# Attention in a fused kernel: six shared PSUM banks, turned groups of a pair in one run, new written-out orders of work

## The chip, the cores and the metric

The kernel runs on one core of a Trainium2 chip. The metric is the device time of one execution in microseconds (us); lower is better.

## What is computed

Three blocks follow one another: windowed attention, a mixture of four attention experts, and a gated block that mixes tokens. The change touches the first and the seam to the second. Cut to what matters:

```python
batch, n_heads, seq, head_dim = (2, 8, 768, 64)
n_sink, window = (4, 128)
scores = scale * np.matmul(q, k.transpose(0, 1, 3, 2))
keep = is_sink | in_window            # in_window: 0 <= i - j < 128
scores = np.where(keep, scores, -1000000000.0)
a = np.exp(scores - np.max(scores, axis=-1, keepdims=True))
a = a / (np.sum(a, axis=-1, keepdims=True) + 1e-09)
x = np.matmul(a, v)                   # then _moe_ref, then _moe2_ref
```

## The kernel before, in words

**Attention.** The 16 heads are worked as 8 pairs. Two heads of a pair lie on the two halves of the partitions, so that the scores of both run side by side in TensorE. The 768 rows of queries are six tiles (t = 0 to 5) of 128. Since the window is 128 wide, a tile meets only its own block of keys, the block before it and the 4 sinks: 260 columns, 132 for tile 0. For each pair and tile these steps follow one another:

- TensorE makes the scores of both heads in two PSUM banks (`score_tile`, L1017).
- VectorE (DVE) adds the mask, takes the row maximum and moves the tile to SBUF in `Pa` (`mask_tile`, L697).
- ScalarE (ACT) takes the exponential and the row sums (`exp_tile`, L511).
- DVE inverts the sums of the whole pair (`invert_sums`, L720 and L722).
- GpSimd (POOL) scales the probabilities in six groups, one for each head h and each group g of two tiles, and gathers the sinks' columns (`scale_pair`, L417 and L419; `gather_sinks`, L428).
- TensorE transposes ("turns") each group into a bank (`turn_group`, L1034; 3 transposes for group 0, 4 for the others) and the gathered sinks (`turn_sinks`, L1048).
- ACT and DVE copy the turned groups to `PTa` (`copy_group`, L521 and L708), three each; DVE copies the sinks (`copy_sinks`, L714).
- TensorE multiplies with the values (`weigh_pair`, L1066) and adds the sinks' part (`weigh_sinks`, L1076), into banks 6 and 7.
- ACT takes the sums out (`take_x`, L529 and L531), DVE the low part (`x_low`, L727).

**Banks.** Scores use banks 0 to 3 (a few tiles of the first pairs banks 4 to 7), turned groups alternate between banks 4 and 5 (`A_TURN`), sums lie in 6 and 7, and the turned sinks in a free part of bank 7.

**Order.** Every engine works its steps in program order and waits on semaphores. The orders are written out in loops at the end of each engine's part. TensorE's loop over pairs p is: scores of pair p+1 tiles 0 and 1, weighing of pair p-1, tiles 2 and 3, sinks of p-1, two turned groups of p, tile 4, two groups, tile 5, two groups, sinks of p turned. In the last pair the first two projections of the experts (`project`, L991 to L993) take the place of tiles 4 and 5, and projections 2 and 3 stand behind the sinks. At the start, `keep_busy` (L1004) multiplies zeros: 9 products before the first scores, 6 before the first turned group.

**POOL and the load queue.** POOL also splits the expert weights into a high and a low part, one strip for each pair (`split_strip`, L405 and L408); its loop is strip, six scalings, gather. All loads are issued by the SyncE queue (SP) in program order: keys and queries of pair p (`load_keys`, L320 and L321), strip p-1 (`load_strip`, L335), values of pair p-1 (`load_values`, L328 and L329). Keys of pair p wait until pair p-2 is scored, values until pair p-3 is weighed. All strips pass through one buffer, `raw[0]`, so the load of strip i waits for both halves of the split of strip i-1:

```python
if i:
    sp.wait_ge(s_["wb_split"], 2 * i)
sp.dma_start(raw[0][:, 0:WB_STEP], w_b[:, i * WB_STEP:(i + 1) * WB_STEP]).then_inc(raw_in[0], 16)
```

After the last pair the orders of the two later stages are as they are; the change does not touch them.

## Time and profile before

| what | us |
|---|---|
| median of three runs | 375.21 (375.20 to 376.01) |
| profiled execution | 375.04 |
| its span, first to last instruction | 373.2 |
| TensorE busy | 365.4 (98%) |
| VectorE, ScalarE, GpSimd busy | 213.5, 191.8, 143.1 |
| granted TensorE clock, mean | 1.00 of full |

The span leaves out what lies ahead of the first and behind the last instruction. Matmuls overlap in the array, so in the timeline the start of the next group says more than a group's length: the time from one start to the next is what a group costs. A number behind x is a count of records; a matmul of float32 data leaves two records, a transpose one. "Idle before" in brackets names what ended an idle stretch. "Pair p's sinks" marks in the timeline of TensorE the transpose of L1048, which ends a pair's block.

### The profile page before, as it was taken

The page shows a single profiled execution, that of the slowest core. Times are in us where ns is not written, and L with a number is a line of the kernel's source. Part 1 is how long each engine was busy: PE and PEld are TensorE (multiplying, and loading weights), DVE is VectorE, ACT ScalarE, POOL GpSimd, SP SyncE. Part 2 cuts the span into 40 slices and gives each one's busy share as a digit, 9 for nine tenths or more (in the row PEclk, how much of TensorE's full clock was granted, in tenths as well). Part 3 has the DMA queues.
Part 4 walks back from the last instruction along what each step waited for, and adds up shares of the span by engine and source line. Part 5 has one row for each costly group of instructions (what it writes and reads, how often), then busy time and mean ns, then how long its engine had stood idle before and what let it go on. Part 6 is the DMA issues. An engine that isn't in the chain of part 4 may idle for free.

```text
span 373.2 us, 7754 instructions
## 1 busy us (share of the span) xinstructions
PE 365.4 (98%) x2854; PEld 334.4 (90%) x2854; DVE 213.5 (57%) x614; ACT 191.8 (51%) x512; POOL 143.1 (38%) x188
## 2 busy tenths in 40 slices
PE   7799999999999999999999999999999999999996
PEld 6577777789998889999988998899999988999996
DVE  3687777632588884068898618633745265325342
ACT  4888888854678782468888353332311033411110
POOL 4898888888746017100455617510000032100000
PEclk9999999999999999999999999999999999999999
DMA  8655555342330000000131201000011200000112
GB/s 251 207 179 189 182 166 180 95 139 83 109 93 2 2 2 2 2 0 3 38 106 35 96 28 56 2 0 2 0 43 44 85 2 0 0 2 0 45 41 85
DMA packets 12885, 24.20 MB, mean 65 GB/s; under 512 B 1328, under 2 KB 6704, under 8 KB 12848
## 3 DMA queue, kind: packets, MB, share of 16 engines
q1 hardware_dynamic: 12848, 23.70, 20.1%
q8 instruction: 23, 0.38, 0.4%
q14 instruction: 14, 0.11, 0.1%
HBM read 20.55 MB, written 3.15 MB: 63 GB/s over the span
## 4 chain that ended last, share of the span: by engine, by line
PE 92%; ACT 3%; POOL 2%; issue 2%; DVE 1%; DVEq 0%; ACTq 0%; POOLq 0%
PE banks L991 15%; PE banks L993 15%; PE banks L992 15%; PE banks L1250 14%; PE banks L1066 5%; PE banks L1034 5%; PE banks L1149 5%; PE banks L1017 5%; PE banks L1185 5%; PE banks L1161 4%; PE banks L1076 2%; ACT Pa L511 2%; POOL Pa L419 1%; PE banks L1004 1%; ACT Pb L577 1%
## 5 line engine op out<-in xcount | busy, mean ns | idle before, releaser
L511 ACT ACTIVATE Pa<-Pa,NMa 128x260 f32<-128x260 f32 (+1 forms) x96 | 46.1, 483 | 12.7 <-DVE NMa L697 12.7
L697 DVE CUSTOM_DVE_ANT_0 Pa<-banks,win 128x260 f32<-128x260 f32 (+1 forms) x96 | 33.6, 402 | 18.0 <-PE banks L1017 18.0
L419 POOL TENSOR_TENSOR Pa<-Pa,RIa 128x520 f32<-128x520 f32 (+1 forms) x48 | 42.3, 912 | 0.0
L492 POOL TENSOR_TENSOR rstd<-vare,minus_half 128x1 f32<-128x1 f32 x12 | 11.9, 990 | 77.6 <-DVE vare L926 77.6
L577 ACT ACTIVATE Pb<-Pb,NM 128x384 f32<-128x384 f32 (+5 forms) x48 | 31.8, 664 | 5.8 <-DVE NM L787 5.4
L677 ACT ACTIVATE gH<-uT 128x384 fp32r<-128x384 f32 x16 | 8.4, 525 | 49.9 <-DVE uT L945 49.9
L787 DVE CUSTOM_DVE_ANT_0 Pb<-banks,causal 128x384 f32<-128x384 f32 (+5 forms) x48 | 28.4, 620 | 7.7 <-PE banks L1149 5.5
L1250 PE MATMUL banks<-w_sgL,vnH 128*128 128x384 f32 x96 | 32.5, 338 | 0.0
L943 DVE TENSOR_TENSOR vb<-banks,b_all 128x384 f32<-128x384 f32 x16 | 8.9, 558 | 37.0 <-PE banks L1250 37.0
L1017 PE MATMUL banks<-kd,qd 64*128 64x260 f32 (+1 forms) x192 | 26.9, 392 | 1.2 <-DMA qd<-in_qT 1.2
L1034 PE MATMUL banks<-ident,Pa 128*128 128x128 f32 x176 | 25.0, 281 | 1.8 <-POOL Pa L419 1.6
L1034 PEld LDWEIGHTS banks<-ident,Pa 128*128 128x128 f32 x176 | 18.8, 141 | 8.6 <-issue 4.9
L643 ACT ACTIVATE V<-banks 128x512 f32<-128x512 f32 x12 | 7.2, 598 | 34.0 <-PE banks L993 29.0
L1161 PE MATMUL banks<-ident,Pb 128*128 128x128 f32 x168 | 23.0, 275 | 0.6 <-ACT Pb L577 0.5
L737 DVE TENSOR_TENSOR ekS<-banks,ekS 64x384 fp32r<-64x384 f32 x16 | 8.8, 551 | 25.2 <-ACT eqH L545 25.1
L924 DVE BATCH_NORM_STATS2 bn<-V 128x6 f32<-128x512 f32 x12 | 8.3, 694 | 25.5 <-ACT V L643 25.5
L1149 PE MATMUL banks<-ekS,eqH 128*128 128x384 f32 (+3 forms) x64 | 21.7, 349 | 0.1
L1161 PEld LDWEIGHTS banks<-ident,Pb 128*128 128x128 f32 x168 | 18.9, 140 | 3.2 <-DVE NM L787 1.6
L992 PE MATMUL banks<-xL,wbH 128*128 128x384 f32 x64 | 21.7, 339 | 0.0
L991 PE MATMUL banks<-gH,w_outH 128*128 128x384 f32 x64 | 21.6, 338 | 0.0
L991 PE MATMUL banks<-xH,wbH 128*128 128x384 f32 x64 | 21.6, 338 | 0.0
L993 PE MATMUL banks<-xH,wbL 128*128 128x384 f32 x64 | 21.6, 338 | 0.0
(153 smaller groups left out, 1075.6 us busy)
## 6 DMA issues: line engine op xcount, KB each, us to landing
va<-in_v SPq DMA_DIRECT2D x8, 384.0 KB, 3.7
out<-raw SPq DMA_DIRECT2D x16, 192.0 KB, 1.9
kd<-in_kT SPq DMA_DIRECT2D x7, 396.0 KB, 3.4
qd<-in_qT SPq DMA_DIRECT2D x7, 384.0 KB, 4.4
vs<-in_vsink SPq DMA_DIRECT2D x8, 336.0 KB, 4.4
raw<-in_w_sgT SPq DMA_DIRECT2D x9, 256.0 KB, 2.7
raw<-in_w_in SPq DMA_DIRECT2D x8, 256.0 KB, 2.7
raw<-in_w_b SPq DMA_DIRECT2D x8, 193.0 KB, 4.7
```

The source lines that it names most:

```text
L419: nc.gpsimd.tensor_tensor(Pa[s][:, h, ts, :], Pa[s][:, h, ts, :], RIa[:, s, h, ts].unsqueeze(2).broadcast_to((P, ts.stop - ts.start, WIN)) ...
L511: nc.scalar.activation(Pa[s][:, h, t, a:WIN], Pa[s][:, h, t, a:WIN], ACT.Exp, bias=NMa[:, s, h, t:t + 1], scale=-1.0, accum_out=RSa[:, s, ...
L577: nc.scalar.activation(Pb[n % DEPTH][:, 0:w], Pb[n % DEPTH][:, 0:w], ACT.Exp, bias=NM[:, e % 2, t:t + 1], scale=-1.0, accum_out=RS[:, e, t ...
L697: nc.vector.tensor_tensor_reduce(out=Pa[s][:, h, t, a:WIN], in0=banks[:, score_bank(p, t) + 2 * (t % 2) + h, 0:WIN - a], in1=m[:, :], scal ...
L991: nc.tensor.matmul(out, aH, bH, start=(n == 0), stop=False)
L992: nc.tensor.matmul(out, aH, bL, start=False, stop=False)
L993: last = nc.tensor.matmul(out, aL, bH, start=False, stop=(n == k - 1))
L1017: last = nc.tensor.matmul(banks[:, score_bank(p, t) + 2 * (t % 2) + h, 0:w], qd[s][half, t * P:(t + 1) * P], kd[s][half, c:c + w], start=T ...
L1034: last = nc.tensor.transpose(banks[:, A_TURN + n % 2, j * P:(j + 1) * P], Pa[p % 2][:, h, t, own * BLK:own * BLK + P], ident[:, :])
L1149: last = nc.tensor.matmul(banks[:, CAUSAL_BANK[t] + i, 0:cols], q[:, e, t * P:(t + 1) * P], ekS[:, e, i * cols:(i + 1) * cols], start=firs ...
L1161: last = nc.tensor.transpose(banks[:, bank, j * P:(j + 1) * P], Pb[n % DEPTH][:, (j0 + j) * P:(j0 + j + 1) * P], ident[:, :])
L1250: last = nc.tensor.matmul(banks[:, T_BANKS[n % 2], 0:HALF], a[:, s, here], x, start=(s == 0 and i == 0), stop=(s == T - 1 and i == 2))
```

## The change

- Banks 0 to 5 are shared by scores, turned groups, turned sinks and the first projections. Which step uses which bank is written in the orders (the last numbers of a token), and a step on TensorE waits for whatever used its bank before (`used_before`, `wait_bank_taken`).
- The orders of TensorE, ACT, DVE and POOL are written out as strings (`A_PE`, `A_ACT`, `A_DVE`, `A_POOL`). The first entry of each is for pair 0, the next for pairs 1 on; TensorE's has two more for the end. Letters: s a score tile (or its mask, or exponential), n the same of the next pair, v a weighed group of the pair before, w its sinks, t a turned group (g.h.bank), c a scaled or copied group, k the sinks, i and j inverted sums (i with a group g in pair 0, j of the next pair), x the sums taken out, l a strip, r a projection.
- In the middle pairs the six turned groups stand in one run, and the weighing is cut in three (group 1; then 2 and 0) with four and two score tiles between.
- ACT copies four turned groups and DVE two (before three each).
- Pair 0: strip 0 is split behind the sinks; sums are inverted for each group. From pair 1 on the strip is first, as before.
- The masks of the attention are made first among POOL's constants and signalled by themselves; the causal mask and the identity follow.
- Seven zero products before the first scores; the six later ones are gone.

Cut to its core:

```diff
-TURNS = [(0, 1, "dve"), (1, 1, "dve"), (0, 0, "act"), (1, 0, "act"), (2, 0, "dve"), (2, 1, "act")]
-TURN_N = len(TURNS)
-A_TURN, A_SUM = 4, 6
+TURN_N = 2 * GROUPS
+A_SUM = 6
...
+A_PE = [order("s0.1.5 s3.3.2 s1.4.0 s2.1.5 s4.3.2 n1.4.0 n2.1.5 s5.0.4 n3.3.2 n5.0.4 n0.1.5 n4.3.2 t1.1.1 t1.0.0 t0.1.3 t2.0.2 k5 t0.0.0 t2.1.4"),
+        order("v1 n0.2.1 n5.4.5 n1.3.0 n2.2.1 v2 v0 n4.2.5 n3.1.0 w t1.1.5 t1.0.4 t0.0.3 t2.0.2 t2.1.5 t0.1.0 k4"),
+        order("v1 v2 v0 w t1.1.4 t1.0.5 r0 t0.0.2 t2.0.3 r1 t2.1.4 t0.1.5 k3"),
+        order("r2 r3 v1 v2 v0 w")]
+A_ACT = [order("s0 s3 s2 s1 s4 n1 s5 n3 n0 n5 n4 n2 c2.1 c0.0"),
+         order("n0 n5 n2 n1 n4 x c1.0 n3 c2.1 c0.0 c0.1")]
+A_DVE = [order("s0 s3 s1 s2 s4 i1 n1 n2 i0 s5 n3 i2 n0 n5 n4 c1.0 c1.1 k c2.0 c0.1 j"),
+         order("n0 n5 n2 n1 n4 n3 c1.1 x c2.0 k j")]
+A_POOL = [order("c1.0 c1.1 c0.0 c0.1 c2.0 c2.1 k l"),
+          order("l c1.1 c1.0 c0.0 c2.1 c2.0 c0.1 k")]
...
+def in_pair(p, steps):
+    shift = {"n": 1, "j": 1, "v": -1, "w": -1, "x": -1}
+    steps = [(step[0], p + shift.get(step[0], 0), *step[1:]) for step in steps]
+    return [x for x in steps if 0 <= x[1] < PAIRS or x[0] == "r"]
+A_PE_STEPS = [x for p, steps in enumerate([A_PE[0]] + [A_PE[1]] * (PAIRS - 2) + A_PE[2:]) for x in in_pair(p, steps)]
+A_ACT_STEPS, A_DVE_STEPS, A_POOL_STEPS = [[x for p in range(PAIRS) for x in in_pair(p, steps[min(p, 1)])] for steps in (A_ACT, A_DVE, A_POOL)]
...
+def used_before(use):
+    k = A_USES.index(use)
+    return ([None] + [what for bank, what in A_USES[:k] if bank == use[0]])[-1]
...
-WARM_UP, WARM_LATER = 9, 6
...
+WARM_UP = 7
...
-                    sp.wait_ge(s_["scored"], T * (p - 1))
+                    sp.wait_ge(s_["scored"], max(A_SCORED[p - 2, t] for t in range(T)))
...
+            nc.gpsimd.memset(win0[:, :], 0.0)
+            nc.gpsimd.memset(win1[:, :], 0.0)
+            step(nc.gpsimd.memset(win[:, :], 0.0))
+            for m in (win0[:, SINK:BLK], win1[:, BLK:WIN], win[:, BLK:WIN]):
...
+            nc.gpsimd.affine_select(out=win1[:, P:BLK], in_=win1[:, P:BLK], compare_op=ALU.is_ge, fill=MASKED, base=0,
+                                    pattern=[[-1, SINK]], channel_multiplier=1).then_inc(s_["consts"], 1)
...
-            nc.gpsimd.memset(win0[:, :], 0.0)
-            nc.gpsimd.memset(win1[:, :], 0.0)
-            nc.gpsimd.memset(win[:, :], 0.0)
             step(nc.gpsimd.memset(causal[:, P:S], 0.0))
...
+            nc.gpsimd.affine_select(out=causal[:, S - P:S], in_=causal[:, S - P:S], compare_op=ALU.is_ge, fill=MASKED, base=0,
+                                    pattern=[[-1, P]], channel_multiplier=1).then_inc(s_["consts"], 1)
...
+            def scale_group(p, g, h):
...
+                pool.wait_ge(s_["sums_inverted"], inverted(p, g))
...
-            for p in range(PAIRS):
-                split_strip(p)
-                scale_pair(p)
-                gather_sinks(p)
+            for what, p, *at in A_POOL_STEPS:
+                if what == "l":
+                    split_strip(p)
+                elif what == "c":
+                    scale_group(p, *at)
+                else:
+                    gather_sinks(p)
...
+            def invert_sums(p, g=None):
                 s = p % 2
-                dve.wait_ge(s_["expd"], 2 * T * (p + 1))
-                nc.vector.tensor_scalar(RIa[:, s, :, :], RSa[:, s, :, :], EPS_SUM, None, ALU.add).then_inc(s_["dve_step"], 1)
-                dve.wait_ge(s_["dve_step"], p + 1)
-                nc.vector.reciprocal(RIa[:, s, :, :], RIa[:, s, :, :]).then_inc(s_["sums_inverted"], 1)
+                ts = slice(0, T) if g is None else slice(2 * g, 2 * g + 2)
+                dve.wait_ge(s_["expd"], 2 * max(A_EXPD[p, t] for t in range(T)[ts]))
+                nc.vector.tensor_scalar(RIa[:, s, :, ts], RSa[:, s, :, ts], EPS_SUM, None, ALU.add).then_inc(s_["dve_step"], 1)
+                dve.wait_ge(s_["dve_step"], inverted(p, g))
+                nc.vector.reciprocal(RIa[:, s, :, ts], RIa[:, s, :, ts]).then_inc(s_["sums_inverted"], 1)
...
+            def wait_bank_taken(use):
+                before = used_before(use)
+                if before is None:
+                    return
+                what, p, *at = before
+                if what == "s":
+                    t, h = at
+                    wait("masked", 2 * A_MASKED[p, t] - 1 + h)
+                elif what == "k":
+                    wait("sinks_in", p + 1)
+                else:
+                    for who, copied in A_COPIED.items():
+                        wait("turned_in_" + who, copied.get(before[1:], 0))
...
+            def turn_group(p, g, h, bank):
+                pe.wait_ge(s_["scaled"], A_SCALED[p, g, h])
+                wait_bank_taken((bank, ("t", p, g, h)))
...
+            def weigh_group(p, g):
...
+                groups = [x[2] for x in A_PE_STEPS if x[:2] == ("v", p)]
+                if g == groups[0]:
+                    pe.wait_ge(v_in[s], 32 * (p // 2 + 1))
+                    wait_sums_taken(p)
+                for who, copied in A_COPIED.items():
+                    wait("turned_in_" + who, max(copied.get((p, g, h), 0) for h in range(2)))
...
+                pe.wait_ge(s_["sinks_in"], p + 1)
...
+                elif b == 0 and n < EARLY_PROJ[0]:
+                    wait_bank_taken((bank, ("r", *[x[1] for x in A_PE_STEPS if x[0] == "r" and x[2] == n], n)))
...
             keep_busy(WARM_UP)
-            for t in range(T):
-                score_tile(0, t)
-            for p in range(PAIRS):
-                if p + 1 < PAIRS:
-                    score_tile(p + 1, 0)
-                    score_tile(p + 1, 1)
-                if p:
-                    weigh_pair(p - 1)
-                if p + 1 < PAIRS:
-                    score_tile(p + 1, 2)
-                    score_tile(p + 1, 3)
-                if p:
-                    weigh_sinks(p - 1)
-                else:
-                    wait("masked", 2 * (T + 2))
-                    keep_busy(WARM_LATER)
-                turn_group(p, 0)
-                turn_group(p, 1)
-                if p + 1 < PAIRS:
-                    score_tile(p + 1, 4)
-                else:
-                    project(0, 0)
-                turn_group(p, 2)
-                turn_group(p, 3)
-                if p + 1 < PAIRS:
-                    score_tile(p + 1, 5)
-                else:
-                    project(0, 1)
-                turn_group(p, 4)
-                turn_group(p, 5)
-                turn_sinks(p)
-            project(0, 2)
-            project(0, 3)
-            weigh_pair(PAIRS - 1)
-            weigh_sinks(PAIRS - 1)
+            for what, p, *at in A_PE_STEPS:
+                if what in "sn":
+                    score_tile(p, *at)
+                elif what == "v":
+                    weigh_group(p, *at)
+                elif what == "w":
+                    weigh_sinks(p)
+                elif what == "t":
+                    turn_group(p, *at)
+                elif what == "k":
+                    turn_sinks(p, *at)
+                else:
+                    project(0, *at)
             for b in range(B):
                 for n in range(EARLY_PROJ[b], PREFIX):
```

## Rows read from the trace of the kernel before

**Rows 1.** The page, part 1: busy us (share of the span) xinstructions, of TensorE.

```profile
PE 365.4 (98%) x2854; PEld 334.4 (90%) x2854; DVE 213.5 (57%) x614; ACT 191.8 (51%) x512; POOL 143.1 (38%) x188
```

**Rows 2.** Table of stretches, pair 1 to pair 6: PE, PEld, DVE, ACT, POOL busy; clock; DMA share; GB/s.

```profile
28.58:76.33 47.75, 47.75 (x577) 36.48 (x576) 34.74 (x154) 40.75 (x142) 40.27 (x56) 1.00 0.53 169
```

**Rows 3.** Timeline of TensorE, one middle pair: start us, length us, engine, line, operation, tiles.

```profile
41.75 1.15 PE L1017 MATMUL banks<-kd,qd 64*128 64x260 f32 x8
...
42.83 0.89 PE L1076 MATMUL banks<-PS,vs 48*64 48x128 f32 x24
...
43.64 0.98 PE L1034 MATMUL banks<-ident,Pa 128*128 128x128 f32 x7
...
44.56 0.71 PE L1017 MATMUL banks<-kd,qd 64*128 64x260 f32 x4
...
45.20 0.98 PE L1034 MATMUL banks<-ident,Pa 128*128 128x128 f32 x7
...
46.75 1.09 PE L1034 MATMUL banks<-ident,Pa 128*128 128x128 f32 x8
...
47.68 0.27 PE L1048 MATMUL banks<-ident,sinks 128*112 128x128 f32 x1
...
47.88 0.93 PE L1017 MATMUL banks<-kd,qd 64*128 64x132 f32 x8
```

**Rows 4.** Timeline of TensorE from the start to the first sinks.

```profile
0.97 4.21 PE L1004 MATMUL banks<-causal 128*128 128x128 f32 x18 [0.97 <-POOL causal L376]
...
5.11 2.69 PE L1017 MATMUL banks<-kd,qd 64*128 64x132 f32 x24
...
9.04 1.81 PE L1017 MATMUL banks<-kd,qd 64*128 64x132 f32 x16 [1.24 <-DMA qd<-in_qT]
...
10.98 1.60 PE L1004 MATMUL banks<-causal 128*128 128x128 f32 x12
...
19.03 0.27 PE L1048 MATMUL banks<-ident,sinks 128*112 128x128 f32 x1
```

**Rows 5.** The chain that ended last (first row), then the timeline of POOL.

```profile
6.12 5.85 ACT Pa L511 x24
...
12.51 0.41 POOL Pa L417
...
18.57 0.27 POOL L428 TENSOR_SCALAR sinks<-Pa 128x96 f32<-128x96 f32 x1
...
18.81 0.83 POOL L405 TENSOR_TENSOR wbH<-raw,ones 128x386 fp32r<-128x386 f32 x1
...
19.72 0.87 POOL L408 TENSOR_TENSOR wbL<-raw,wbH 128x386 fp32r<-128x386 f32 x1
```

**Rows 6.** Timeline of the load queue, then the loads of the strips' buffer.

```profile
11.80 0.33 SPq L335 DMA_DIRECT2D raw<-in_w_b  x1
...
DMA to landing us min/median/max: 3.3/4.7/6.3
```

**Rows 7.** Groups by shape, 29 to 76 us: xcount, busy us, mean ns, idle before.

```profile
L511 ACT ACTIVATE Pa<-Pa,NMa 128x260 f32<-128x260 f32 x50 | 24.9, 500 | 5.7 <-DVE NMa L697 5.7
...
L511 ACT ACTIVATE Pa<-Pa,NMa 128x132 f32<-128x132 f32 x10 | 4.0, 398 | 1.2 <-DVE NMa L697 1.2
...
L521 ACT ACTIVATE PTa<-banks 128x512 f32<-128x512 f32 x10 | 5.9, 587 | 0.0
...
L521 ACT ACTIVATE PTa<-banks 128x384 f32<-128x384 f32 x5 | 2.5, 491 | 0.1
...
L529 ACT ACTIVATE xH<-banks 128x768 fp32r<-128x768 f32 x3 | 2.4, 788 | 0.0
```

**Rows 8.** Timeline of TensorE: sinks of pairs 6 and 7.

```profile
76.33 0.27 PE L1048 MATMUL banks<-ident,sinks 128*112 128x128 f32 x1
...
85.25 0.27 PE L1048 MATMUL banks<-ident,sinks 128*112 128x128 f32 x1
```

More of the change, by code:

```diff
@@ new lines, with counted @@
+A_ACT_STEPS, A_DVE_STEPS, A_POOL_STEPS = [[x for p in range(PAIRS) for x in in_pair(p, steps[min(p, 1)])] for steps in (A_ACT, A_DVE, A_POOL)]
+def counted(steps, letters, keep=4):
+    return {x[1:keep]: n + 1 for n, x in enumerate([x for x in steps if x[0] in letters])}
+A_SCORED, A_MASKED, A_EXPD = [counted(x, "sn", 3) for x in (A_PE_STEPS, A_DVE_STEPS, A_ACT_STEPS)]
+A_TURNED, A_SCALED = counted(A_PE_STEPS, "t"), counted(A_POOL_STEPS, "c")
+A_COPIED = {"act": counted(A_ACT_STEPS, "c"), "dve": counted(A_DVE_STEPS, "c")}
@@ new lines, with inverted, bank_uses, score_banks @@
+A_INVERTED = counted(A_DVE_STEPS, "ij", 3)
+def inverted(p, g):
+    return A_INVERTED.get((p, g), A_INVERTED.get((p,)))
+def bank_uses(step):
+    if step[0] in "sn":
+        return [(bank, ("s", *step[1:3], h)) for h, bank in enumerate(step[3:])]
+    return [(step[-1], step[:-1])] if step[0] in "tk" else [(PROJ_BANKS[0][step[2]], step)] if step[0] == "r" else []
+A_USES = [use for step in A_PE_STEPS for use in bank_uses(step)]
+def score_banks(p, t):
+    return next(x[3:] for x in A_PE_STEPS if x[0] in "sn" and x[1:3] == (p, t))
@@ L115 @@
              [("kq", e, 1) for e in range(E)] + [("v", 4, 1), ("v", 5, 1), ("v", 3, 1)]
-WARM_UP, WARM_LATER = 9, 6
-def score_bank(p, t):
-    return 4 if (p, t // 2) in ((0, 1), (1, 0)) else 0
-def masks_ahead(p, t):
-    k = T * p + t
-    if k < 4:
-        return 0
-    return 2 * (k - 3 if k < 2 * T - 2 else k - 1)
-def copies_by(who, g):
-    return [sum(w == who for _, _, w in TURNS[:n + 1]) for n, (group, _, w) in enumerate(TURNS) if group == g and w == who]
+WARM_UP = 7
 MIXES = [(g, m) for g in range(2) for m in range(KT)]
@@ L778, in mask_causal @@
                 e, t = divmod(n, T)
+                wait("consts", 2 if b == 0 else 0)
                 wait("e_scored", E * T * b + SCORED[n])
@@ L1033, in turn_group @@
                         continue
-                    last = nc.tensor.transpose(banks[:, A_TURN + n % 2, j * P:(j + 1) * P], Pa[p % 2][:, h, t, own * BLK:own * BLK + P], ident[:, :])
+                    last = nc.tensor.transpose(banks[:, bank, j * P:(j + 1) * P], Pa[p % 2][:, h, t, own * BLK:own * BLK + P], ident[:, :])
                 last.then_inc(s_["turned"], 1)
@@ L1115, in project @@
                         wait("proj_low", 2 * E * b + sum(k != "v" for k, _, _ in PROJ_ORDER[:m + 1]))
-                elif b == 0 and bank < 4:
-                    wait("masked", 2 * T * PAIRS)
+                elif b == 0 and n < EARLY_PROJ[0]:
+                    wait_bank_taken((bank, ("r", *[x[1] for x in A_PE_STEPS if x[0] == "r" and x[2] == n], n)))
                 elif b == 0 and bank < 6:
-                    wait("turned_in_act", GROUPS * PAIRS)
-                    wait("turned_in_dve", GROUPS * PAIRS)
+                    for who, copied in A_COPIED.items():
+                        wait("turned_in_" + who, max(copied.values()))
+                    wait("sinks_in", PAIRS)
                 elif b == 0:
```

154 lines of the change are left out of this document (58 added, 96 removed).

## Prediction

> **What bounds the kernel now.** I read the shares of busy time first: TensorE is at work for 365.4 of 373.2 us [rows 1], so the question is where its time goes, not whether something else is slow. Then the table of stretches: from the sinks' transpose of pair 1 to that of pair 6, TensorE is busy 47.75 of 47.75 us at a granted clock of 1.00, while ACT has 40.75 and POOL 40.27 [rows 2]. In the middle of the attention stage TensorE alone sets the pace: one pair per 9.55 us (19.03 to 47.68 is three pairs [rows 3, 4]). Before pair 0's sinks are turned it is another picture: TensorE waits for keys and queries, then for POOL's scaled groups [rows 4, 5], and the chain of the end runs through ACT's exponentials [rows 5]. So two things can be won here: shorter TensorE work per pair, and an earlier first pair. After the last weighing the two kernels are the same and TensorE-bound, so what stands at the end of attention stands at the end of the kernel.
>
> **Fewer changes of kind.** TensorE's steps are of four kinds with different tile shapes: scores (64x128), weighing (128x64), sinks (48x64), transposes (128x128). Rows 3 price a change. Eight transposes take 0.93 us and seven followed by scores 0.92; a transpose followed by scores 0.20. With p for one transpose, e for entering a run and x for leaving it: 8p+e = 0.93, 7p+e+x = 0.92, p+x = 0.20, so p = 0.11, x = 0.10, e = 0.06. Two score tiles take 1.08 us to the next kind, one tile 0.64: a tile is 0.44, entering and leaving 0.20. So a lone score tile between two pairs of turned groups costs 0.20 + 0.10 + 0.06 = 0.36 us beyond its work: 0.18 a change. A pair before has nine changes (s v s w t s t s t and back); the new order v n v n w t has six. Three fewer are worth 3 x 0.18 to 3 x 0.20 = 0.54 to 0.60; I take 0.56, period 8.99 us. The work itself (matmuls, transposes, copies, their bytes) is the same. The five periods between pair 1's and pair 6's sinks give 5 x 0.56 = 2.8 us. Pair 7's block has no scores (8.92 us, 76.33 to 85.25 [rows 8]) and gains nothing.
>
> **Do the others keep up with 8.99?** ACT gets one more copy of 384 columns and DVE gives it up. By full durations ACT's pair is 10 x 0.50 + 2 x 0.40 + 2 x 0.59 + 2 x 0.49 + 0.79 = 8.75 us [rows 7], an upper bound, since its instructions overlap by about 0.1 each. POOL: 12.51 to 18.57 is six scalings (6.06), 0.24 for the sinks, and a strip 0.91 + 0.87 with 0.1 between [rows 5], 8.2 in all. DVE has less. The six groups are turned in one run at the block's end; each copy is due only when its group is weighed in the next block, two kinds later. Six banks for scores and turned groups instead of four and two add no wait that I find in the middle pairs. I cost the new bank waits there at nothing, covered by that order; if ACT's cover fails, rival C prices it.
>
> **The start.** Masks' constants are done first on POOL, so DVE is not held by them; the first scores need only the first pieces of keys and queries. Seven instead of nine zero products (18 records in 4.21 us, 0.23 each [rows 4]; four fewer) free TensorE about 0.9 us earlier, but the second tile (3) waits for the second pieces, which in the kernel before were in by the third tile at 5.67 at the latest. So masks flow hardly earlier. The gain is in the order behind: before, the sums of pair 0 are inverted after all of pair 0's exponentials (6.12 + 5.85 = 12.0) and POOL starts at 12.51 [rows 5]; now group 1 (tiles 2 and 3) is inverted alone after six exponentials, 2 x 0.40 + 4 x 0.50 = 2.8 us from about 6.2, with some 0.3 of waiting for masks: POOL starts at about 9.5. Its scalings take 6.06 and two short waits for the inverses of groups 0 and 2 (0.2), so the sinks are gathered at 15.8, against 18.57: 2.8 us earlier. The six zero products that go (10.98 to 12.4 [rows 4]) stood in idle time and are worth nothing by themselves.
>
> **The wait that is added.** The strip of the expert weights moves. Before, strip 0 is split at 9.85, ahead of the scaling, while POOL has nothing else, and the load of strip 1 is issued at 11.80, as soon as the split lets the buffer go [rows 5, 6]. Now strip 0 is split behind pair 0's sinks and strip 1 right behind it, "strip first" in pair 1. Both use one buffer, and SP issues load 1 only on the second increment of strip 0. So POOL splits strip 0 from 16.0 to 17.9, load 1 is issued at 17.9, and POOL stands, with all of pair 1's scaling queued behind. How long is in the rows: strips take 3.3 us at least, 4.7 in the median and 6.3 at most from issue to landing [rows 6]; the 3.3 is that of strip 1 itself, with no keys just ahead of it, as it will be here; later ones go out behind keys. I take 3.4, a touch more for the values and keys that SP issues right behind. POOL goes on at 21.3, splits strip 1 until 23.2, scales pair 1 for 6.06 until 29.2 (the last group turned is the last scaled), and 0.4 later the sinks of pair 1 are turned: 29.6, against 28.58 before. TensorE's own work for pair 1, weighing pair 0 and scoring pair 2, is done at about 23.3 (16.1, 0.8 for two groups of pair 0 still to turn, 6.4 for the block up to its transposes), and it waits in between. The early start of 2.8 us and the saved 0.56 are gone, and 1.0 more. Behind load 1 SP holds values 1 and keys 3; issued by 21, they are needed from 29.7 on: covered. Later strips are again issued a pair ahead.
>
> **The end.** In the last block projection 2 needs bank 2, which holds turned group (0, head 0) of pair 7. ACT copies it after group (2, head 1), whose transposes come only behind projection 1. Sinks turned, then two copies of 0.5 finish: projection 2 waits about 0.8 us. That is new.
>
> **Sum** at projection 2, where the kernel before stands at 85.3: 29.6 + 5 x 8.99 + 8.92 + 0.8 = 84.3. So -1.0 us. Against the profiled execution, 375.04 us (span 373.2, 1.8 around it), that is 374.0; the median of the runs is 0.17 above the profiled one, so 374.2.
>
> **Rivals.**
> A, as summed. Its bounds: strip 1 at 3.3 to 4.7 us (-0.1, +1.3), the start 0.5 either way, changes at 0.20 (-0.2), the wait at the end gone (-0.8). Own range 372.6 to 376.0; 0.66.
> B, the strip does not hold pair 1 (it lands in time, or POOL's lateness is taken up by TensorE's own work). Then POOL scales pair 1 from 19.8 to 25.9 and the stage ends 2.9 earlier: 371.3. For it: now POOL has 7.5 us of room in five pairs [rows 2]. Against: the increment that SP waits for comes after POOL's own last step. 0.10.
> C, slower: ACT becomes the bound. It is idle 7.0 us in five pairs now, 1.4 each [rows 2]; with 0.49 more work and the same idle time a pair would take 10 us. The idle time is slack that TensorE leaves, so I expect it to shrink to 0.3; but copies now all stand behind the one run of transposes, and the first weighing waits for two of them. It decides from 0.24 us of idle time by durations, about 0.4 by starts. At 0.8 of idle time the period is 9.55 again, all 2.8 us are gone: 377.0. 0.12.
> The Trainium skill ("TensorEngine Tiling (Array Packing)", PSUM Bottleneck) says that speeding up TensorE leaves PSUM evacuation as it was and the copy may become the bound. By that rule C is what happens; the room in rows 2 and 7 speaks against it.
> D, the clock. The zero products at the start took 0.23 us a record, the later ones 0.13 (1.60 for 12) [rows 4]: half rate (1.2 GHz) and full (2.4). TensorE then stood still 1.24 us before 9.04 and scores went on at full rate. The new order leaves idle stretches of 0.4 to 1.7 us between 4.8 and 12.3 with fewer products in them. If the first scores stay at half rate it costs 0.5 us; if the clock falls again in block 1, 22 transposes at 0.11 and part of the weighing double and some 2 us are lost beyond what the wait for POOL hides: 374.7 to 376.2. 0.12.
> The Trainium skill ("TensorE: Matmul & The Clock Gate", A second HAM failure mode: psum-queue depth-cycling) tells of a kernel whose short idles between groups, cycling through banks, let the clock swing. By that rule D is the case; nothing in the trace before swings.
>
> **Numbers.** The bound of faster and slower is 0.3%, 1.1 us, about what a measurement of this kernel can tell from no change. A: 0.24 faster, 0.38 same, 0.04 slower. B: 0.10 faster. C: 0.03 same, 0.09 slower. D: 0.09 same, 0.03 slower. Together 0.34, 0.50, 0.16. The range 372.6 to 376.3 leaves out B and the greater part of C.
>
> **What would show it.** Sinks of pair 0 turned near 16.1; POOL idle over 3 us before the split of strip 1, at 17.9 to 21.3; sinks of pair 1 near 29.6; then 8.99 a pair with no wait of TensorE; ACT's idle time near 0.3 a pair; a wait of 0.8 before projection 2. B falls if the idle stretch is there and pair 1 is late; C falls with a period of 9.0; D shows in the spacing of scores of pairs 0 and 1. My forecast is wrong in kind if pair 1's sinks come before 28, or if the period is not within 0.1 of 8.99.

## The result, and the profile after

Over 20 executions each, the changed kernel takes 377.14 us in the median (376.18 to 379.98) and the kernel before 375.55 (374.60 to 376.53): ratio 1.0051, 95% interval 1.0035 to 1.0067. It is slower by 0.5%, and outside the range of the forecast (374.2, 372.6 to 376.3). The profiled execution took 377.40 us.

The page of the changed kernel, span and part 1; the columns are those of [rows 1]:

```profile
span 375.6 us, 7796 instructions
PE 363.9 (97%) x2838; PEld 334.5 (89%) x2838; DVE 212.2 (56%) x612; ACT 193.3 (51%) x518; POOL 143.0 (38%) x188
```

TensorE works 1.5 us less than in [rows 1], and the span is 2.4 us longer: waits have come in. Where, a ledger of TensorE's timeline shows (us from the span's start; the forecast beside it):

| start of | before | forecast | after | forecast missed by, step by step |
|---|---|---|---|---|
| pair 0's sinks | 19.03 | 16.1 | 16.54 | +0.4 |
| pair 1's sinks | 28.58 | 29.6 | 31.08 | +1.0 |
| pair 6's sinks | 76.33 | 74.55 | 77.51 | +1.5 (five periods) |
| pair 7's sinks | 85.25 | 83.5 | 86.42 | 0.0 |
| projection 2 | 85.28 | 84.3 | 87.32 | +0.1 |
| first projection after the last weighing | 92.38 | | 94.44 | |

The changed kernel stands 2.1 us behind the old one where the two become alike, and at projection 2 it stands 3.0 behind the forecast. At the end of the span it is 2.4 behind (375.6 against 373.2): another 0.3 us arises in the later stages, which the forecast took as the same. The same 0.3 is lost there with the new order in x1_strip (0.77 ahead at projection 2, 0.5 at the end); I have no cause for it.

The table of stretches from pair 1's sinks to pair 6's, columns as in [rows 2]:

```profile
31.08:77.51 46.43, 46.43 (x577) 37.15 (x576) 32.89 (x148) 41.27 (x144) 40.60 (x56) 0.99 0.46 147
```

Five periods take 46.43 instead of 47.75 us: 9.29 each (9.24 once the first is past) instead of 9.55, where 8.99 was forecast. ACT has 41.27 of it: 5.16 us idle, 1.0 a pair. It is not the bound.

POOL's timeline (start, length, line, tiles; in brackets the idle time before, and what ended it), then the load queue's and the loads of the strips' buffer:

```profile
9.43 2.07 POOL L469 TENSOR_TENSOR Pa<-Pa,RIa 128x520 f32<-128x520 f32 x2 [4.42 <-DVE RIa L765]
...
16.21 0.27 POOL L478 TENSOR_SCALAR sinks<-Pa 128x96 f32<-128x96 f32 x1
...
17.36 1.01 POOL L459 TENSOR_TENSOR wbL<-raw,wbH 128x386 fp32r<-128x386 f32 x1
21.86 0.83 POOL L456 TENSOR_TENSOR wbH<-raw,ones 128x386 fp32r<-128x386 f32 x1 [3.49 <-DMA raw<-in_w_b]
```
```profile
18.40 0.33 SPq L385 DMA_DIRECT2D raw<-in_w_b  x1
...
DMA to landing us min/median/max: 3.4/4.8/6.0
```

This is the chain as it was forecast: scaling from 9.43 (9.5), sinks gathered at 16.21 (15.8), the load of strip 1 issued at 18.40 (17.9), POOL idle for 3.49 (3.4). What the forecast did not have is in TensorE's timeline of that stretch and the table of stretches around it (the seventh column after the times is the granted clock):

```profile
24.70 0.66 PE L1079 MATMUL banks<-ident,Pa 128*128 128x128 f32 x4 [0.49 <-POOL Pa L469]
...
28.68 2.61 PE L1079 MATMUL banks<-ident,Pa 128*128 128x128 f32 x11 [1.48 <-POOL Pa L469]
31.08 0.42 PE L1093 MATMUL banks<-ident,sinks 128*112 128x128 f32 x1
31.43 1.15 PE L1110 MATMUL banks<-PTa,va 128*64 128x128 f32 x16
```
```profile
20.00:25.00 5.00, 4.51 (x67) 3.37 (x68) 3.45 (x20) 4.84 (x21) 3.06 (x4) 1.00 0.97 296
25.00:30.00 5.00, 2.88 (x17) 2.17 (x16) 1.72 (x3) 1.99 (x6) 4.91 (x9) 0.82 1.02 296
30.00:35.00 5.00, 5.00 (x50) 3.74 (x50) 2.60 (x13) 2.83 (x10) 4.48 (x6) 0.84 0.39 130
35.00:40.00 5.00, 5.00 (x74) 4.27 (x71) 3.94 (x18) 4.85 (x17) 4.83 (x8) 1.00 0.08 15
```

TensorE waits 2.6 us for POOL in four stretches, and the clock goes from 2.4 to 1.2 GHz for some of this time. The eleven last transposes take 2.40 us (28.68 to 31.08, 0.22 each) where fifteen took 1.63 in a kernel without that wait (x1_strip below, 0.11 each). In 16 of the 20 executions the mean clock is 0.995 or less, in the kernel before it is 0.999 or 1.000 in 25 of the 27 executions taken beside the first four experiments.

One middle pair of TensorE, to be laid beside [rows 3]:

```profile
49.77 0.27 PE L1093 MATMUL banks<-ident,sinks 128*112 128x128 f32 x1
49.98 1.09 PE L1110 MATMUL banks<-PTa,va 128*64 128x128 f32 x16
51.00 2.06 PE L1067 MATMUL banks<-kd,qd 64*128 64x132 f32 x16
52.99 1.75 PE L1110 MATMUL banks<-PTa,va 128*64 128x128 f32 x28
54.67 1.15 PE L1067 MATMUL banks<-kd,qd 64*128 64x260 f32 x8
55.74 0.89 PE L1121 MATMUL banks<-PS,vs 48*64 48x128 f32 x24
56.56 2.62 PE L1079 MATMUL banks<-ident,Pa 128*128 128x128 f32 x22
59.02 0.27 PE L1093 MATMUL banks<-ident,sinks 128*112 128x128 f32 x1
```

Six changes of kind, and the 22 transposes take 2.46 us up to the sinks, as p and e of the prediction have it (22 x 0.11 + 0.06 = 2.48). Only the run of four score tiles is too long: 51.00 to 52.99 is 1.99 us, where 4 x 0.44 less 0.22 for tile 0's one block of keys and 0.20 for the changes make some 1.74. The 0.25 over is the whole difference between 9.24 and 8.99. The fourth tile of the run (tile 2, `n2.2.1`) goes into the banks of the first (tile 0, `n0.2.1`). DVE's timeline:

```profile
51.68 0.29 DVE L740 CUSTOM_DVE_ANT_0 Pa<-banks,win 128x132 f32<-128x132 f32 x1 [0.96 <-PE banks L1067]
51.90 0.08 DVE L740 DVE_READ_ACCUMULATOR2_ANT NMa<- 128x1 f32 x1
51.90 0.29 DVE L740 CUSTOM_DVE_ANT_0 Pa<-banks,win 128x132 f32<-128x132 f32 x1
52.12 0.08 DVE L740 DVE_READ_ACCUMULATOR2_ANT NMa<- 128x1 f32 x1
```

By single records tile 0's last score ends at 51.49, its first mask starts 0.19 later, the second one's maximum is read until 52.20, and tile 2 starts at 52.35; scores are 0.22 apart, so without a wait it would start at 52.21. That is 0.14 lost. The other 0.11 are in tile 2's own two passes: 0.29 from the first to the second, and 0.35 to the next kind, instead of 0.22 and 0.31.

The seam to the experts, TensorE's timeline:

```profile
86.42 0.27 PE L1093 MATMUL banks<-ident,sinks 128*112 128x128 f32 x1
87.32 0.39 PE L1025 MATMUL banks<-wbH,xH 128*128 128x260 f32 x1 [0.63 <-ACT PTa L573]
```

0.90 us from the sinks to projection 2, where the ledger has 0.03 before (85.25 to 85.28).

### The profile page after: what moved, and what is told of

Read it like the earlier page. It is cut to its first block, busy times and chain, and to the rows that moved or that the text cites. A ratio compares the mean times of both kernels' runs of the same rounds, so it can differ in the third digit from the quotient of the medians.

```text
span 375.6 us, 7796 instructions
## 1 busy us (share of the span) xinstructions
PE 363.9 (97%) x2838; PEld 334.5 (89%) x2838; DVE 212.2 (56%) x612; ACT 193.3 (51%) x518; POOL 143.0 (38%) x188
## 4 chain that ended last, share of the span: by engine, by line
PE 88%; POOL 3%; DMA 2%; DVE 2%; issue 2%; ACT 2%; SPq 1%; DVEq 0%; ACTq 0%; POOLq 0%
PE banks L1025 15%; PE banks L1027 15%; PE banks L1026 15%; PE banks L1296 13%; PE banks L1195 5%; PE banks L1231 5%; PE banks L1110 5%; PE banks L1079 5%; PE banks L1067 4%; PE banks L1207 4%; POOL Pa L469 2%; PE banks L1121 2%; DMA qd<-in_qT 1%; DMA raw<-in_w_b 1%; ACT Pb L620 1%
## 5 line engine op out<-in xcount | busy, mean ns | idle before, releaser
L1067 PE MATMUL banks<-kd,qd 64*128 64x260 f32 (+1 forms) x192 | 25.7, 386 | 3.2 <-DVE NMa L740 1.6
L1079 PE MATMUL banks<-ident,Pa 128*128 128x128 f32 x176 | 23.6, 286 | 3.0 <-POOL Pa L469 2.6
L1079 PEld LDWEIGHTS banks<-ident,Pa 128*128 128x128 f32 x176 | 20.1, 146 | 5.8 <-POOL Pa L469 4.3
L1067 PEld LDWEIGHTS banks<-kd,qd 64*128 64x128 f32 x192 | 15.8, 186 | 10.1 <-issue 7.2
L1110 PE MATMUL banks<-PTa,va 128*64 128x128 f32 x352 | 22.4, 277 | 0.0
L1110 PEld LDWEIGHTS banks<-PTa,va 128*64 128x64 f32 x352 | 19.0, 137 | 3.7 <-issue 3.7
```

The costliest lines, as they stand in the source:

```text
L1067: last = nc.tensor.matmul(banks[:, bank, 0:w], qd[s][half, t * P:(t + 1) * P], kd[s][half, c:c + w], start=True, stop=True)
L1079: last = nc.tensor.transpose(banks[:, bank, j * P:(j + 1) * P], Pa[p % 2][:, h, t, own * BLK:own * BLK + P], ident[:, :])
L1110: nc.tensor.matmul(banks[h * D:(h + 1) * D, A_SUM + t // G3, at], va[s][:, h, key, :], PTa[:, h, blk * P:(blk + 1) * P], start=(opens and ...
```

## The experiments

Each is the changed kernel with one edit, unless it says more. "Sinks" are the starts of the sinks' transpose; medians, ranges and numbers of executions are given, and the ratio is to the kernel before on the same chip. Beside x1 to x4 the kernel before took 375.26 us (27 executions), beside y1 to y5 375.32 (14), beside z1 to z4 375.30 (11); beside the changed kernel it had taken 375.55. So a difference of 0.3 us from the changed kernel's 377.14 is no more than what the kernel before shows between such groups. Where the diffs below show one order only, the orders of the other engines were changed to match.

### x1_strip: strip 0 first in pair 0, as before the change

```diff
-A_POOL = [order("c1.0 c1.1 c0.0 c0.1 c2.0 c2.1 k l"),
+A_POOL = [order("l c1.0 c1.1 c0.0 c0.1 c2.0 c2.1 k"),
```

> Edit: in pair 0 POOL splits strip 0 first, as in the kernel before; all else as changed. Theory (the new wait for strip 1 costs pair 1 about 2.9 us, and TensorE's idle stretches in it let the clock fall, another 1.2): POOL no longer idles before strip 1's split, granted clock 1.00 through pair 1, sinks of pair 1 near 26 to 27 instead of 31.1, time about 3 to 4 us below the changed kernel, near 373.5. Rival (the strip's wait is taken up by work that is late anyway, the loss sits in the middle pairs): sinks of pair 1 stay at 29 or later and the time stays within 1 us of the changed kernel's.

374.46 us (373.30 to 374.63, 10), ratio 0.9970 [0.9958, 0.9981]: 2.7 us below the changed kernel. Timelines of POOL and TensorE:

```profile
18.32 0.83 POOL L456 TENSOR_TENSOR wbH<-raw,ones 128x386 fp32r<-128x386 f32 x1
19.22 0.87 POOL L459 TENSOR_TENSOR wbL<-raw,wbH 128x386 fp32r<-128x386 f32 x1
20.54 2.06 POOL L469 TENSOR_TENSOR Pa<-Pa,RIa 128x520 f32<-128x520 f32 x2 [0.45 <-DVE RIa L765]
```
```profile
26.83 1.80 PE L1079 MATMUL banks<-ident,Pa 128*128 128x128 f32 x15
28.46 0.27 PE L1093 MATMUL banks<-ident,sinks 128*112 128x128 f32 x1
```

Strip 1 is there when POOL comes to it. From pair 0's sinks (18.41) to pair 1's (28.46) are 10.05 us instead of 14.54, though pair 0's come 1.9 later. With the wait goes the fall of the clock (0.999 or 1.000 in nine of ten executions).

### z1_twobuf: the same wait taken away in another way

Odd strips land in the second buffer, which attention leaves idle; the order is the changed one.

```diff
-                if i:
-                    sp.wait_ge(s_["wb_split"], 2 * i)
-                sp.dma_start(raw[0][:, 0:WB_STEP], ...).then_inc(raw_in[0], 16)
+                if i > 1:
+                    sp.wait_ge(s_["wb_split"], 2 * (i - 1))
+                sp.dma_start(raw[i % 2][:, 0:WB_STEP], ...).then_inc(raw_in[i % 2], 16)
```

> Edit: the order stays as changed (strip 0 behind pair 0's sinks, strip 1 first in pair 1), but odd strips get the second buffer, which is idle until the last pair, so that load 1 does not wait for the split of strip 0. Theory (it is the one shared buffer that makes POOL stand 3.5 us, and that idle time which lets the clock fall): no idle time before strip 1's split, sinks of pair 0 still near 16.5, sinks of pair 1 near 27, granted clock 1.00, time 3 to 4 us below the changed kernel, 373.1 to 374.1. Rival (what helped in the run with strip 0 first was the later start of pair 0, not the missing wait): pair 1's sinks at 29 or later, time above 375.5.

373.84 us (373.13 to 373.92, 4), ratio 0.9958 [0.9944, 0.9971]. POOL's timeline:

```profile
18.59 1.01 POOL L459 TENSOR_TENSOR wbL<-raw,wbH 128x386 fp32r<-128x386 f32 x1
19.55 0.84 POOL L456 TENSOR_TENSOR wbH<-raw,ones 128x386 fp32r<-128x386 f32 x1
```

No idle time between the strips, pair 0's sinks at 17.77 and pair 1's at 27.83. So it is the one buffer, not the place of the split, that made the wait: 3.3 us of the median.

### x2_fill: the clock kept up through the wait

While TensorE waits for POOL in pair 1 it multiplies zeros into the bank of the next group: 3, 2, 2 and 8 products ahead of groups (1,1), (1,0), (0,0) and (2,0). They change no result. The wait for the bank is moved ahead of the wait for POOL, so that the zeros can go in.

```diff
+                fills = {(1, 1, 1): 3, (1, 1, 0): 2, (1, 0, 0): 2, (1, 2, 0): 8}
...
+                for _ in range(fills.get((p, g, h), 0)):
+                    nc.tensor.matmul(banks[:, bank, 0:P], causal[:, 0:P], causal[:, 0:P], start=True, stop=True)
```

> Edit: the strip stays as changed, but in pair 1 TensorE multiplies zeros (3, 2, 2 and 8 products) into the next group's own bank while it waits for POOL. Theory (idle TensorE in pair 1 is what lets the clock fall to half): granted clock 1.00 everywhere, the last eleven transposes of pair 1 at 0.11 us apart instead of 0.21, sinks of pair 1 near 29.9 instead of 31.1, time 1 to 1.3 us lower. Rival (the clock fell for another reason, or its fall was hidden in the wait for POOL): clock below 1.00 again, or sinks of pair 1 at 31 with the clock at 1.00; time unchanged.

376.87 us (376.35 to 377.33, 6), ratio 1.0035 [1.0020, 1.0049]. The clock stays at 0.998 to 1.000 in all six. TensorE's timeline:

```profile
28.44 1.95 PE L1076 MATMUL banks<-causal 128*128 128x128 f32 x16
30.22 1.36 PE L1082 MATMUL banks<-ident,Pa 128*128 128x128 f32 x11
31.42 0.27 PE L1096 MATMUL banks<-ident,sinks 128*112 128x128 f32 x1
```

Eleven transposes take 1.20 us again, and from pair 0's sinks (17.97) to pair 1's it is 13.45 instead of 14.54 us. But this 1.1 is not the clock's. Strip 1 landed sooner in this execution: POOL's idle time was 2.57 us, not 3.49. From the split of strip 1 (22.37) to the sinks it is 9.05 us, where the changed kernel has 9.22 (21.86 to 31.08). What the clock gave, the zero products took. POOL's timeline:

```profile
22.37 0.83 POOL L456 TENSOR_TENSOR wbH<-raw,ones 128x386 fp32r<-128x386 f32 x1 [2.57 <-DMA raw<-in_w_b]
26.49 2.64 POOL L469 TENSOR_TENSOR Pa<-Pa,RIa 128x260 f32<-128x260 f32 x3
```

Group (2, head 0) was scaled at 29.13, and TensorE came to it at 30.22, when its eight products were through: 1.1 us late. Pair 0 was 1.4 late besides (its first scores ran at half rate), and the median gains 0.3. So this run shows that zero products keep the clock up, but not what its fall costs.

### z4_allfill: the clock kept up in pair 0 as well

Zero products also ahead of tiles of the start (4, 2, 4) and of the first turned group (1), and fewer in pair 1 (2, 1, 1, 6).

```diff
+            early = {("s", 1, 1): 4, ("s", 0, 5): 2, ("s", 1, 5): 4, ("t", 0, 1, 1): 1}
...
+                keep_busy(early.get(key, 0))
```

> Edit: the changed kernel with zero products in all idle places: 4, 2, 4 and 1 in pair 0 (ahead of the scores of pair 1 tile 1, pair 0 tile 5, pair 1 tile 5, and the first turned group) and 2, 1, 1 and 6 in pair 1. Theory (the removed products and the new idle time cost clock, by chance in place and length): mean granted clock 0.998 or more in every execution where the changed kernel had 0.995 or less in 16 of 20, no time above 378, median 0.5 to 1 us lower, 376.1 to 376.6. Rival (the clock's fall lies inside the wait for POOL and costs nothing in the median): clock at 1.00, median 377.0 as before.

376.96 us (376.06 to 378.12, 4), ratio 1.0055 [1.0037, 1.0073]; clock 0.997 to 1.000. In the profiled execution sinks stand at 16.71 and 29.22 and projection 2 at 85.26, 2.1 us ahead of the changed kernel; 1.0 of it is that strip 1 landed sooner (POOL idle for 2.46 us). The medians do not show this: the median span is 374.6 against 375.35, and up to 2.5 us lie outside the span against 1.8 (I have no reason for it). Here the zero products were over in time: from the split of strip 1 (21.01) to the sinks it is 8.21 us instead of 9.22. So the clock's fall is real and costs 1.0 us in pair 1 (y1_warm, next, says the same without zero products there); it is not what decides between 374 and 377 in the median. With the strip's wait gone (z1_twobuf) it needs no zero products.

### y1_warm: nine zero products at the start again

```diff
-WARM_UP = 7
+WARM_UP = 9
```

> Edit: nine zero products at the start instead of seven; the six later ones stay gone. In the traces so far the changed kernel and its variants showed the scores of the start at 0.22 us a pass in four executions and at 0.43 until about 9 us in two, and their times spread over nearly 4 us. Theory (with seven products TensorE is idle from 4.7 to 5.2 or 5.8 us, while the clock is still at half, and whether it rises then is chance): with nine products the first scores start at about 5.1 and run on at 0.22 a pass every time, sinks of pair 0 near 16.5, the times above 378 vanish and the median falls by 0.3 to 0.8 us. Rival (the spread comes from the clock's fall in pair 1 and from the loads, which this does not touch): spread and median as for the changed kernel, 377.1.

377.07 us (376.27 to 377.66, 7), ratio 1.0045 [1.0028, 1.0061]; clock 0.995 in all. The theory fell: the first scores still came at half rate until about 6.6, and a later run of scores did too. TensorE's timeline:

```profile
13.38 2.54 PE L1067 MATMUL banks<-kd,qd 64*128 64x260 f32 x12 [1.29 <-DVE NMa L740]
```

(twelve records in 2.5 us; the changed kernel has x12 in 1.41). Here the clock fell in pair 0, behind waits of 0.66 us for queries and 0.70 and 1.29 for masks: it is 0.50 from 13.40 to 16.80. In pair 1 TensorE waited for POOL as before, and it stayed at 1.00:

```profile
29.27 1.49 PE L1079 MATMUL banks<-ident,Pa 128*128 128x128 f32 x11 [1.48 <-POOL Pa L469]
30.60 0.30 PE L1093 MATMUL banks<-ident,sinks 128*112 128x128 f32 x1
```

From the split of strip 1 (22.45) to the sinks it is 8.15 us, against 9.22 with the fall in pair 1: the cleanest price of the fall there, 1.07 us. The same mean of 0.995 can stand for a fall in either place. The number of products at the start does not decide it; what does is not shown.

### x3_maskwait: the mask's wait for its scores ahead of its other waits

```diff
+                dve.wait_ge(s_["scored"], A_SCORED[p, t])
                 if p >= 2:
...
-                dve.wait_ge(s_["scored"], A_SCORED[p, t])
```

> Edit: in the mask step the wait for the scores is named first, so that it can sit in the mask instruction itself, and the two waits for the pair two before behind it. Theory (each middle pair loses 0.26 us because tile 2's scores want tile 0's banks back, and DVE's first mask starts 0.18 us after the scores' end, 0.13 of it a separate wait): first mask of a pair about 0.1 earlier, the period 9.24 falls to 9.10 to 9.18, 0.4 to 0.7 us in all. Rival (the 0.26 is no bank wait but a price of the four-tile run): period unchanged at 9.24.

376.61 us (375.68 to 378.42, 10), ratio 1.0044 [1.0027, 1.0060]; the period is 9.11. TensorE's timeline of a middle pair:

```profile
50.60 1.92 PE L1067 MATMUL banks<-kd,qd 64*128 64x132 f32 x16
52.45 1.75 PE L1110 MATMUL banks<-PTa,va 128*64 128x128 f32 x28
```

1.85 instead of 1.99. As changed, the wait for the scores came last of three, and a separate wait instruction stood between semaphore and mask (51.55, the mask at 51.68). With the order turned, that instruction is through before the scores end, and tile 2 starts without delay (51.81, 0.22 behind the pass before it). TensorE follows DVE's first step by the full 0.14, so the loss is the bank's reuse. What is left, 0.11 a pair, is that tile 2's passes still stand 0.29 and 0.35 apart.

### y4_banks: the reused bank moved away

Three and three score tiles instead of four and two, so that each tile finds its bank long free.

```diff
-        order("v1 n0.2.1 n5.4.5 n1.3.0 n2.2.1 v2 v0 n4.2.5 n3.1.0 w t1.1.5 t1.0.4 t0.0.3 t2.0.2 t2.1.5 t0.1.0 k4"),
+        order("v1 n0.1.2 n5.0.3 n1.4.5 v2 v0 n2.1.2 n4.0.3 n3.4.5 w t1.1.2 t1.0.1 t0.0.3 t2.0.0 t2.1.4 t0.1.5 k1"),
```

> Edit: tile 2 of the next pair's scores is moved behind weighed groups 2 and 0, so that runs of three and three tiles use six banks each and no run wants back a bank that its own first tile has filled; banks renumbered to fit, masks and exponentials in the same order as the scores. Changes of kind stay at six. Theory (0.26 us a pair is the wait for tile 0's masks inside the four-tile run): period 8.99 to 9.08, 0.9 to 1.4 us less in all. Rival (another wait, on the copies or on the masks before the first turned group, takes its place): period 9.15 or more.

377.27 us (376.04 to 378.91, 7), ratio 1.0053 [1.0035, 1.0072]; the period is 9.38, longer by 0.14. TensorE's timeline:

```profile
49.46 0.28 PE L1093 MATMUL banks<-ident,sinks 128*112 128x128 f32 x1
49.92 1.09 PE L1110 MATMUL banks<-PTa,va 128*64 128x128 f32 x16 [0.18 <-DVE xL L770]
50.94 1.50 PE L1067 MATMUL banks<-kd,qd 64*128 64x132 f32 x12
52.37 1.75 PE L1110 MATMUL banks<-PTa,va 128*64 128x128 f32 x28
```

The first run of scores still has some 0.13 too much (1.43 for 3 x 0.44 - 0.22 + 0.20 = 1.30), and a new wait stands ahead of the weighing: banks 6 and 7 are not yet read by `x_low`, which DVE now reaches later. The wait went from one shared bank to another.

### y3_split: a lone score tile back between the turned groups

```diff
-        order("... v2 v0 n4.2.5 n3.1.0 w t1.1.5 t1.0.4 t0.0.3 ..."),
+        order("... v2 v0 n4.2.5 w t1.1.5 t1.0.4 n3.1.0 t0.0.3 ..."),
```

> Edit: in the middle pairs tile 3 of the next pair's scores is moved into the run of turned groups, behind its second group (and DVE's order to match); two changes of kind more in a pair, the same work. Theory (a change of kind costs 0.18 us): period of 9.24 becomes 9.60, 2.1 us more in all, near 379.3. Rival (the change of kind is hidden, or the copies and masks that the split lets start earlier pay for it): period stays at 9.24 to 9.4. If it is well over 9.6, a wait has come in on top, which the first transposes behind the tile will show.

379.98 us (379.47 to 380.48, 4), ratio 1.0122 [1.0104, 1.0139]; the period is 10.17. TensorE's timeline:

```profile
56.41 1.06 PE L1079 MATMUL banks<-ident,Pa 128*128 128x128 f32 x8 [0.30 <-DVE NMa L740]
57.40 0.71 PE L1067 MATMUL banks<-kd,qd 64*128 64x260 f32 x4
58.04 1.75 PE L1079 MATMUL banks<-ident,Pa 128*128 128x128 f32 x14
```

Of the 0.93 that a pair grows, 0.36 are two more changes of kind, as priced (57.40 to 58.04 is the 0.64 of a lone tile). The rest are waits: 0.37 ahead of the first turned group (55.22 to 56.41 is 1.19, where the changed kernel has 0.82), which the trace puts down to masks for 0.30, and 0.21 ahead of the weighing (0.43 from the sinks, where the changed kernel has 0.21). So the price of a change holds, and the order around it has no slack for a tile that comes late.

### x4_endcopy: ACT copies (0, head 0) ahead of (2, head 1) in the last pair

```diff
+A_ACT.append(order("x c1.0 c0.0 c2.1 c0.1"))
```

> Edit: in the last pair ACT copies group (0, head 0) before group (2, head 1). Theory (projection 2 waits 0.6 to 0.8 us for bank 2): the wait goes, projection 2 starts right behind the last sinks, time 0.6 to 0.8 us lower. Rival (the next thing, the copy of group 2 or bank 3, is late instead and takes the wait over): time unchanged within 0.2 us in the trace.

376.09 us (375.43 to 377.91, 10), ratio 1.0025 [1.0009, 1.0041]. TensorE's timeline:

```profile
85.67 0.27 PE L1094 MATMUL banks<-ident,sinks 128*112 128x128 f32 x1
85.70 0.37 PE L1026 MATMUL banks<-wbH,xH 128*128 128x260 f32 x1
```

The wait ahead of projection 2 is gone (0.87 us), and the median is 1.05 lower. Strip 1 also landed sooner in the profiled execution (POOL idle for 2.44 us), so its 375.50 us shows more than this edit.

### y5_best, z2_best42, z3_besttwo: the mended parts together

y5_best has x1_strip, x3_maskwait, x4_endcopy, y1_warm and y4_banks; z2_best42 only the first three, in the run of four tiles as changed; z3_besttwo two buffers (z1_twobuf) with x3_maskwait and x4_endcopy.

> Edit: all that helped together: strip 0 first, nine zero products, three and three tiles, the scores' wait named first in the mask step, ACT's order in the last pair. Theory (the parts add: pair 1's sinks near 28.3 or earlier, five periods of 9.0, no wait before projection 2): five to six us below the changed kernel, near 371.6 to 372.4, and some 3 us below the kernel before. Rival (the parts share one slack, POOL or ACT becomes the bound at 9.0): period over 9.1 and time above 373.

> Edit: strip 0 first in pair 0, scores' wait first in the mask step, ACT's order at the end; runs of four and two tiles as changed. Theory (parts add where they lie in different places): pair 1's sinks near 28.4, period 9.11, no wait before projection 2: 1.5 us below the run with strip 0 first alone (374.5), near 373.0. Rival: the period falls back to 9.24 or the end's wait returns, time 374 or more.

> Edit: two strip buffers with the order of strips as changed, scores' wait first, ACT's order at the end. Theory: the early start of pair 0 (16.5) is kept and not paid back, pair 1's sinks near 27, period 9.11, no wait at the end: near 371.5 to 372.3, the lowest of all. Rival (the loads, now issued closer together, delay keys or values): a wait for a load on TensorE in pairs 1 to 3, time above 373.

| kernel | median (range, executions) | ratio to before | period | pair 1's sinks | projection 2 |
|---|---|---|---|---|---|
| y5_best | 373.34 (372.56 to 373.91, 6) | 0.9944 [0.9930, 0.9959] | 9.24 | 27.22 | 82.53 |
| z2_best42 | 372.08 (371.86 to 372.30, 5) | 0.9915 [0.9903, 0.9927] | 9.11 | 27.47 | 81.94 |
| z3_besttwo | 372.45 (371.02 to 372.93, 6) | 0.9916 [0.9899, 0.9933] | 9.11 | 27.88 | 82.38 |

z2_best42 beats both kernels, by 3.2 us (0.85%) and, measured apart, 5.1. y5_best missed its range as its rival has it, and its period of 9.24 says again that three and three tiles are the worse order. z3_besttwo had no earlier pair 0 to show for its freer order: its first scores ran at half rate, as did those of z2_best42. TensorE's timeline of the start, first z2_best42, then the changed kernel:

```profile
5.27 4.96 PE L1068 MATMUL banks<-kd,qd 64*128 64x260 f32 x24 [0.20 <-DMA qd<-in_qT]
```
```profile
5.21 2.40 PE L1067 MATMUL banks<-kd,qd 64*128 64x260 f32 x16 [0.45 <-DMA qd<-in_qT]
```

24 records in 4.96 us against 16 in 2.40 is not the difference of work alone: single records start 0.43 us apart until about 9 in the one and 0.22 in the other.

## Why the prediction was wrong, by its own steps

- **The early start**: right in kind and near in size. Forecast 16.1, came 16.54. That it came so near is in part luck: of the ten profiles with strip 0 behind pair 0's sinks this one is the earliest, the others have 16.57 to 18.00.
- **The wait that is added**: right in mechanism and place (3.49 us of idle time for 3.4). The tenth is luck: the other seven profiles with this wait have 2.44 to 3.24 us, all below the 3.3 that the prediction took as the least. Rival B is false. x1_strip and z1_twobuf take it away in two ways and win 2.7 and 3.3 us.
- **Fewer changes of kind**: right. The block shows six changes at the price of [rows 3], and y3_split's two more cost 0.36.
- **The step that failed** is the one on the banks: "Six banks for scores and turned groups instead of four and two add no wait that I find in the middle pairs. I cost the new bank waits there at nothing, covered by that order". They cost 0.25 us a pair, 1.3 in five pairs: almost half of the 2.8 that was to be won. The cover named was that of the copies, two kinds later, and for those it holds. The masks were not looked at. Tile 2 takes tile 0's banks after only two other tiles, which leave 0.72 us from tile 0's end to where tile 2 could start (51.49 to 52.21). In this time lie 0.19 for DVE to start, 0.52 for two masks of a short tile and 0.15 for TensorE to start again: 0.86, too long by 0.14. x3_maskwait takes this half of the loss away; the other 0.11, slower passes behind the bank's wait, no row of before shows.
- **Put at nothing in the sum, and as large: the clock.** Rival D was given 0.12 and taken as a case by itself, at some 2 us; it came on top of A. TensorE waits for POOL in four stretches (that followed from the forecast's own step), and there the clock falls: 1.0 us in pair 1 and 0.2 behind it in the profiled execution. By these prices either term alone, the banks or the clock, would have left the time inside the range.
- **The clock in the median and in the spread.** In the median it is smaller: the four changed executions at 1.000 took 376.56 to 377.17, the thirteen at 0.995 have a median of 377.24, and both kernels with zero products in the waits stay near 377. Nor does the mean clock explain the spread, 3.8 us against 1.9 before. The two longest executions (379.63 and 379.98) have 0.991 and 0.986, but another at 0.991 took 376.55, and those at 0.995 run from 376.18 to 378.94. The profiles show two other things that vary from one execution to the next: pair 0's sinks by 1.5 us and strip 1's wait by 1.0.
- **What lets the clock fall.** The Trainium skill ("TensorE: Matmul & The Clock Gate", A second HAM failure mode: psum-queue depth-cycling) has short idles between groups let the clock swing. The trace agrees in part: the clock falls where TensorE stands still between groups. But in the middle pairs, with banks cycled just so, it stays at 1.00, and not every wait brings a fall (y1_warm's pair 1 has 1.48 us of it at 1.00). In the profiles the falls stand behind waits for another engine or a load, not with the cycling; which wait brings one is not shown.
- **ACT the bound (rival C)**: its number, 377.0, was hit for another reason. ACT has 1.0 us a pair idle, and no wait of TensorE in the middle pairs ends with it. It is busy for 8.25 us a pair, below the 8.75 of the prediction. By the Trainium skill ("TensorEngine Tiling (Array Packing)", PSUM Bottleneck) the copy out of PSUM may become the bottleneck. The trace agrees only in part: a read of PSUM does hold TensorE, but by the latency of tile 0's two masks on DVE, not by the load of the copying engine.
- **The end**: right (0.90 for 0.8), and x4_endcopy takes it away.

The sum again with what was measured: +0.4 start, +1.0 clock in pair 1, +1.3 banks, +0.2 clock behind it, +0.1 end, 3.0 us from the forecast's 84.3 to 87.3. In the medians it is 2.9 (377.14 for 374.2), of which 0.3 is that the kernel before itself took 375.55 in the 20 executions, and not the 375.21 that the forecast started from.

Open: why the zero products of z4_allfill bring so little in the median though its profiled stretch shortens by 1.0 us; where the 0.3 us behind the seam comes from; where the clock falls and why; and what decides whether the first scores run at 1.2 or 2.4 GHz until 9 us.

## What to carry to other kernels

When two loads of one buffer are moved to stand back to back on the engine that empties it, the load's whole latency becomes a stall; put the second load in another buffer, or leave something between. Price each reused bank by its own chain, from the writer's last step over the reader's start, its whole work and the writer's restart, against the work that stands between the two uses; that there are more banks than before says nothing of it. And a wait moved from one bank to the next is still a wait: time each order of tiles before it is taken. Zero products that keep the clock up through a wait have to end before what is waited for arrives, and a single profile of a wait for a load can be 1 us off the next: before an edit is credited with a shorter stretch, see whether its load came sooner.

## What was not expected of the hardware

- A mask whose wait for scores stands last among several semaphores starts 0.19 us behind the last score, 0.13 of it a separate instruction; moving that one wait to the front shortens each pair by 0.13 us (9.24 to 9.11).
- Two passes of scores that come behind a bank's wait stand 0.29 and 0.35 us apart instead of 0.22 and 0.31, even where the wait ended in time.
- What the clock does at the start does not follow the idle time ahead of the second pieces of keys: with 0.2 to 0.7 us of it, five of the twelve experiments' profiles (x1_strip, x2_fill, z1_twobuf, z2_best42, z3_besttwo) show scores at 0.43 us apart until about 9 us, the others at 0.22 from 5.2 to 6.6 on, x3_maskwait with 1.12 us of it among them. With strip 0 behind the sinks it goes with a later pair 0 (sinks at 17.77 in z1_twobuf, 16.54 in the changed kernel). With strip 0 first it is hardly worth anything: y5_best has scores at 0.22 from the start and pair 0's sinks at 17.41, z2_best42 at 17.55. So z3_besttwo may have this left, z2_best42 hardly.
- The clock fell behind 2.6 us of waiting in four pieces (up to 1.48) in the profiled execution, and the mean clock says that it fell somewhere in 16 of 20. In y1_warm it fell in pair 0, behind waits of 0.66, 0.70 and 1.29 us, and not in pair 1.
- The same load of strip 1, issued at the same step, lets POOL go on after 2.44 to 3.49 us, in eight profiles.
